# Joining the first 32-wide inverse on TensorE, with the second pair's transposes and gram products moved between the chain's stages

## What is computed

```python
k_n = k / (np.linalg.norm(k, axis=-1, keepdims=True) + 1e-06)
for t in range(S):
    y[:, :, t] = einsum('bhd,bhde->bhe', q[:, :, t], state)
    v_old = einsum('bhde,bhd->bhe', state, kt)
    state = state + bt * einsum('bhd,bhe->bhde', kt, vt - v_old)
x = y.transpose(0, 2, 1, 3).reshape(B * S, H * D)
x = (x @ w_a) * (x @ w_b) @ w_out
h = x @ w_in
out = (np.maximum(h, 0) + alpha * np.minimum(h, 0)) @ w_out2
```

## Time and profile before

| | us |
|---|---|
| median of 3 runs (lowest, highest) | 1044.02 (1043.78, 1046.03) |
| the profiled execution | 1043.06 |
| its span, first to last instruction | 1041.3 |

### The profile page before, as it was taken

How to read it: one execution, slowest core, us unless ns; L and a number is a source line. 1 busy time by engine, 2 the same in 40 slices (tenths; PEclk the granted TensorE clock), 3 DMA queues, 4 the chain that set the end, 5 groups by cost and what they waited for, 6 DMA issues and landing times.

```text
span 1041.3 us, 23976 instructions
## 1 busy us (share of the span) xinstructions
PE 1015.5 (98%) x10049; PEld 854.4 (82%) x10049; DVE 573.2 (55%) x891; ACT 405.9 (39%) x772; POOL 121.3 (12%) x126
## 2 busy tenths in 40 slices
PE   7779999999999999999999999999999999999998
PEld 6557888898888888787889788889888888888898
DVE  6967866554686343486444477544368633322433
ACT  3516445564314344413444422435431333321433
POOL 4324663450000010000001000001000000000000
PEclk9799999999999999999999999999999999999999
DMA  8827998787985566786557596556556445766662
GB/s 117 170 61 246 314 322 276 244 273 240 233 225 165 164 187 195 198 243 182 148 154 248 152 257 194 157 169 199 181 169 195 153 140 184 232 194 194 184 191 80
DMA packets 191738, 203.80 MB, mean 196 GB/s; under 512 B 109232, under 2 KB 139168, under 8 KB 191632
## 3 DMA queue, kind: packets, MB, share of 16 engines
q1 hardware_dynamic: 189040, 200.92, 65.5%
q0 software_dynamic: 896, 1.01, 0.5%
q10 hardware_dynamic: 1696, 0.34, 0.2%
HBM read 166.04 MB, written 31.46 MB: 190 GB/s over the span
## 4 chain that ended last, share of the span: by engine, by line
PE 93%; DVE 4%; issue 1%; ACT 1%; DMA 1%; POOL 0%; SPq 0%; DVEq 0%; ACTq 0%; POOLq 0%
PE bank L508 28%; PE bank L510 27%; PE bank L509 27%; PE bank L625 2%; PE bank L728 1%; PE bank L647 1%; PE bank L672 1%; PE bank L678 1%; PE bank L675 1%; PE bank L693 1%; PE bank L537 1%; PE bank L570 1%; PE bank L722 1%; PE bank L725 1%; DMA k_tok<-in_k_dram 1%
## 5 line engine op out<-in xcount | busy, mean ns | idle before, releaser
L961 ACT CAST g_hi<-g_sb 128x512 fp32r<-128x512 f32 x168 | 104.2, 620 | 246.1 <-DVE g_sb L1242 154.8
L508 PE MATMUL bank<-x_hi,w_two 128*128 128x512 f32 x432 | 171.5, 397 | 1.0 <-DVE x_lo L1231 1.0
L1247 DVE SCALAR_TENSOR_TENSOR g_sb<-f_sb,neg_alpha,e_sb 128x512 f32<-128x512 f32 x96 | 73.7, 768 | 177.5 <-ACT f_sb L958 176.9
L509 PE MATMUL bank<-x_lo,w_two 128*128 128x512 f32 x432 | 168.7, 391 | 0.0
L510 PE MATMUL bank<-x_hi,w_two 128*128 128x512 f32 x432 | 168.7, 391 | 0.0
L1253 DVE TENSOR_TENSOR g_lo<-g_sb,g_hi 128x512 fp32r<-128x512 f32 x168 | 121.1, 721 | 79.4 <-ACT g_hi L961 79.1
L510 PE MATMUL bank<-w_two,g_lo 128*128 128x384 f32 x384 | 129.5, 337 | 0.0
L508 PE MATMUL bank<-w_two,g_hi 128*128 128x384 f32 x384 | 129.4, 337 | 0.0
L509 PE MATMUL bank<-w_two,g_hi 128*128 128x384 f32 x384 | 129.0, 336 | 0.0
L1242 DVE TENSOR_TENSOR g_sb<-e_sb,bank 128x512 f32<-128x512 f32 x72 | 49.5, 687 | 136.0 <-PE bank L510 135.6
L508 PE MATMUL bank<-m_hi,w_two 128*128 128x512 f32 x288 | 118.2, 411 | 0.1
(11 more groups left out here) (153 smaller groups left out, 1543.0 us busy)
## 6 DMA issues: line engine op xcount, KB each, us to landing
w_two<-split_scratch SPq DMA_DIRECT2D x340, 384.0 KB, 3.5
split_scratch<-w_two SPq DMA_DIRECT2D x68, 384.0 KB, 4.5
w_ring<-in_moe_w_out_dram SPq DMA_DIRECT2D x28, 192.0 KB, 4.5
q_tok<-in_q_dram SPq DMA_DIRECT2D x24, 192.0 KB, 4.8
out_dram<-o_sb SPq DMA_DIRECT2D x24, 192.0 KB, 3.6
k_tok<-in_k_dram SPq DMA_DIRECT2D x23, 192.0 KB, 4.7
w_ring<-in_moe_w_in_dram SPq DMA_DIRECT2D x16, 192.0 KB, 4.2
x_raw<-y_sb SPq DMA_DIRECT2D x30, 96.0 KB, 2.4
```

The costliest lines, as they stand in the source:

```text
L508: pe.matmul(dst, lhs_hi, rhs_hi, start=start, stop=False)
L509: pe.matmul(dst, lhs_hi, rhs_lo, start=False, stop=False)
L961: act.copy(g_hi[:, j % GR], g_sb[:, j % GR]).then_inc(gh_ok, 1)
L1247: dve.scalar_tensor_tensor(g_sb[:, j % GR], f_sb[:, f % 2], neg_alpha[:, f:f + 1], e_sb[:, f % 2], ALU.mult, ALU.add).then_inc(g_ok, 1)
```

## The change

- The first inverse (pair 0) stops after the blocks of 16. A transpose X0 of half the columns goes to `dgc`, whose other half POOL has set to zero; JY multiplies it on TensorE by the gram blocks (128 products of 32 x 32 by 32 columns into banks 0 and 1), ACT copies the result to `below` (which is `prod`); JZ multiplies that by the transposed upper blocks (128 products, 16 columns); JF subtracts it in `xt` on DVE, in two parts. The transpose XT0 of the whole stands ahead of JZ. Later pairs keep the old solver.
- TR and GG of pair 1 get banks 2 and 3 of a pool of four. TR 6 and 7 and the four sets of GG move between the stages of chunks 0 and 1.
- Fillers: five, three and two around pair 0's first transposes instead of three; none between the stages up to H3 of chunk 1.
- TRK 3 and the norms (KP, KN, KI) go ahead of all four GK; BP 1 ahead of TRQ 2.
- `k_raw` of pair 1 is loaded from POOL's queue behind VS; the weights' first load waits for JF 0; the x loads are dealt out anew; GM, SQ 3, KS 3, KN 1 and KI 1 come later; the second pair's DG and solver start one unit later.

```diff
-        att, y0_bank, g0_bank = bank[6:8], bank[2:4], (bank[1], bank[4], bank[5], bank[3])
-        spare, kn_bank, b0_bank = (bank[0], bank[2]), bank[3], bank[5]
+        ab = (bank[6], bank[7], bank[0], bank[2])
+        att, y0_bank, g0_bank = ab[0:2], bank[3:5], (bank[1], bank[4], bank[5], bank[3])
+        kn_bank, b0_bank, jz_bank = bank[3], bank[5], (bank[3], ab[3])
...
-        seq += [("F", 3)] * 3 + [("KS0", 0), ("KS0", 1), ("TRK", 0), ("TRK", 1), ("TRK", 2), ("BP", 0), ("GK", 0, 0)]
-        seq += [("KS0", 2), ("KS0", 3), ("TRK", 3), ("KP",), ("KN", 0), ("KI", 0), ("GK", 1, 0), ("GK", 0, 1), ("GK", 1, 1)]
+        seq += [("F", 3)] * 5 + [("KS0", 0), ("KS0", 1), ("TRK", 0)] + [("F", 3)] * 3 + [("TRK", 1)] + [("F", 3)] * 2
+        seq += [("KS0", 2), ("KS0", 3), ("TRK", 2), ("TRK", 3), ("BP", 0), ("KP",), ("KN", 0), ("KI", 0)]
+        seq += [("GK", 0, 0), ("GK", 1, 0), ("GK", 0, 1), ("GK", 1, 1)]
...
-        for g in TR_ORDER:
-            seq += [("TR", 1, g)] + [("F", 3)] * (2 * (g >= 4))
-        for g in range(2):
-            for c in (2, 3):
-                seq += [("GG", c, g)]
-        seq += [("SQ", 2)]
-        for n in range(1, ROWS + 1):
+        seq += [("TR", 1, g) for g in TR_ORDER[0:6]]
+        for n in range(1, R16 + 1):
             seq += [("ROW", 0, n)]
-        seq += [("XT", 0)] + [("F", 0, R16 + 14)] * 3 + [("F", 0, ROWS)]
-
-        seq += [("PT", 0, 0, 0), ("PT", 0, 1, 0)]
...
+        seq += [("X0",), ("JY",), ("XT0",), ("PT", 0, 0, 0), ("PT", 0, 1, 0), ("PT", 0, 1, 1), ("JZ",), ("JF", 0), ("JF", 1)]
+
+        beside0 = {(0, "H2"): [("GG", 2, 0)], (0, "H3"): [("TR", 1, 6)], (0, "H4"): [("TR", 1, 7)],
+                   (0, "HY"): [("XL", 0, 0, T)], (1, "H1"): [("GG", 3, 0), ("PT", 1, 0, 0), ("WS", 0)],
+                   (1, "H2"): [("GG", 2, 1), ("PT", 1, 1, 0), ("WS", 1)],
+                   (1, "H3"): [("GG", 3, 1), ("PT", 1, 1, 1), ("WS", 2)],
+                   (1, "H4"): [("SQ", 2), ("KS", 2), ("WS", 3), ("WT", 0), ("WT", 1)]}
...
-                seq += [(kind, c)] + [("F", 0, 1)] * (3 * (c > 0 or kind not in ("HS", "HY"))) + beside0.get((c, kind), [])
+                seq += [(kind, c)] + [("F", 5)] * (3 * (c > 0 and kind in ("H4", "HY", "HS"))) + beside0.get((c, kind), [])
...
+        X_SP, X_ACT, X_POOL = (0, 3, 8), (1, 4), (2, 5, 6, 7, 9)
...
+                    if n == 0:
+
+                        sp.wait_ge(solve, NSOL0 - 1)
...
+                elif kind == "JY":
+
+                    pe.wait_ge(gk_free, 4)
+                    pe.wait_ge(dz_ok, 1)
+                    pe.wait_ge(solve, R16 + 2)
+                    for b in range(2):
+                        bk = in_bank(b, *st)
+                        for w in range(U):
+                            for i in range(4):
+                                mm = pe.matmul(bk[quad(i), SB * w:SB * w + SB], gs(b)[quad(i), w, SB * (i % 2):SB * (i % 2) + SB],
+                                               dgc[quad(i), U * b + w, :], start=True, stop=True)
+                        mm.then_inc(full[b], 1)
+                elif kind == "JZ":
+
+                    pe.wait_ge(gc_ok, 1)
+                    pe.wait_ge(solve, R16 + 3)
+                    for b in range(2):
+                        pe.wait_ge(*is_free(b, "JY"))
...
+                        for w in range(U):
+                            n = U * b + w
+                            for i in range(4):
+                                mm = pe.matmul(jz_bank[b][quad(i), BB * w:BB * w + BB], below[quad(i), n, :],
+                                               xt[quad(i), n, BB:SB], start=True, stop=True)
+                        mm.then_inc(jz_full, 1)
...
+                elif kind == "JY":
+                    for b in range(2):
+                        act.wait_ge(*is_full(b, *st))
+                        act.copy(below[:, U * b:U * b + U].rearrange("p w i -> p (w i)"), att[b][:, :]).then_inc(free[b], 1)
...
+                elif kind == "JF":
+                    some = slice(U * st[1], U * st[1] + U)
+                    dve.wait_ge(jz_full, st[1] + 1)
+                    dve.wait_ge(solve, R16 + 3)
+                    dve.tensor_tensor(xt[:, some, BB:SB], xt[:, some, BB:SB],
+                                      jz_bank[st[1]][:, 0:U * BB].rearrange("p (n i) -> p n i", i=BB), ALU.subtract).then_inc(solve, 1)
...
+            pool.wait_ge(solve, 1)
+            pool.memset(dgc[:, :, BB:SB], 0.0).then_inc(dz_ok, 1)
...
+                elif kind == "LK" and st[1] == 1:
+                    load_k(pool, 1, st[2], k1_ld)
```

More of the change, by code:

```diff
@@ L118, in build @@
         prod = sb("prod", [P, 2, EB * EB * EB])
+        below = prod[:].rearrange("p a b -> p (a b)").rearrange("p (n i) -> p n i", i=SB)
         mid = sb("mid", [P, 2 * EB * EB])
@@ L141, in build @@
         sq_ok, ks_ok, kn_ok, n_ok, ki_ok, v_ok = (sem(n) for n in ("sq_ok", "ks_ok", "kn_ok", "n_ok", "ki_ok", "v_ok"))
-        full, free = [sem("full0"), sem("full1")], [sem("free0"), sem("free1")]
+        full, free = [sem(f"full{b}") for b in range(4)], [sem(f"free{b}") for b in range(4)]
         y0_full, y0_free = sem("y0_full"), sem("y0_free")
         sq0_ok, ks0_ok, kp_full, b_full, b_ok = (sem(n) for n in ("sq0_ok", "ks0_ok", "kp_full", "b_full", "b_ok"))
-        sp_full, sp_free, su_ok = sem("sp_full"), sem("sp_free"), sem("su_ok")
-        sw_ok, dgp_ok = sem("sw_ok"), sem("dgp_ok")
+        su_ok, sw_ok, dgp_ok, dz_ok, jz_full = (sem(n) for n in ("su_ok", "sw_ok", "dgp_ok", "dz_ok", "jz_full"))
         gk_full, gk_free, gq_full, pt0_ok = sem("gk_full"), sem("gk_free"), sem("gq_full"), sem("pt0_ok")
@@ L263, in tile_units @@
+        seq += [("XL", 0, T, P), ("LV", 2), ("LV", 3), ("WT", 2)] + [("F", 5)] * 10 + [("XS", 0, kc) for kc in range(KC)] + [("HE", 1), ("SQ", 3), ("KS", 3), ("KN", 1), ("KI", 1)]
         def tile_units(i):
@@ L287, in beside @@
             else:
+                at[0].append(("GM", 2))
+                at[1].append(("GM", 3))
                 at[35].append(("PM", 2))
@@ L383, in build @@
         NX = len(list(x_parts()))
-        XP = [[sum(1 for n, x in enumerate(x_parts()) if x[2] == kc and (n % 3 == 2) == gp) for kc in range(KC)] for gp in range(2)]
+        X_SP, X_ACT, X_POOL = (0, 3, 8), (1, 4), (2, 5, 6, 7, 9)
+        XP = [[sum(1 for n, x in enumerate(x_parts()) if x[2] == kc and (n in X_POOL) == gp) for kc in range(KC)] for gp in range(2)]
         def x_rows(queue, p, lo, hi, some, loaded):
             yv = y_sb[:].rearrange("p (b u) s -> p b u s", b=B)
-            for h, e, kc, row, n in list(x_parts())[some]:
+            for h, e, kc, row, n in [list(x_parts())[m] for m in some]:
                 queue.dma_start(x_raw[row:row + n, kc].rearrange("p (b s) -> p b s", b=B)[:, :, lo:hi],
@@ L492, in _ @@
                         sp.wait_ge(unit_ok, NU * (p - 1) + last_ab + 1)
-                    x_rows(sp, p, lo, hi, slice(0, NX), x_ld)
+                    x_rows(sp, p, lo, hi, range(NX), x_ld)
                 elif kind == "OS":
@@ L608, in _ @@
                     for i in (2 * g, 2 * g + 1):
-                        pe.wait_ge(*is_free(i % 2, "TR", p, i))
-                        pe.wait_ge(*is_free(i % 2, "TR", p, 4 + i))
-                    if c == 3:
-                        if g == 0:
-                            pe.wait_ge(b_ok, 2)
-                        else:
-                            pe.wait_ge(sp_free, 2)
-                        bk, filled = spare, (sp_full, sp_full)
-                    else:
-                        bk, filled = in_banks(*st), full
+                        pe.wait_ge(*is_free(tr_bank(p, i), "TR", p, i))
+                        pe.wait_ge(*is_free(tr_bank(p, i), "TR", p, 4 + i))
+                    if (c, g) == (2, 0):
+                        pe.wait_ge(solve, NSOL0)
+                    two = (2, 3) if c < 4 else (0, 1)
+                    bk = [in_bank(b, *st) for b in two]
                     for j in range(UQ):
@@ L1119, in _ @@
                     dve.wait_ge(consts, MASKS)
-                    if c == 3:
-                        dve.wait_ge(sp_free, 4)
-                    else:
-                        for hf in range(2):
-                            dve.wait_ge(*is_free(hf, "GG", c, 1))
+                    for hf in range(2):
+                        dve.wait_ge(*is_free(2 + hf, "GG", c, 1))
                     dve.tensor_tensor(pt(c)[:], pt(c)[:], upper[:, 0].unsqueeze(1).to_broadcast([P, UH, T]), ALU.mult)
```

121 lines of the change are left out of this document (64 added, 57 removed).

## The result

The changed kernel takes 1048.35 us (median of five runs, 1048.1 to 1049.85). Beside it the kernel before took 1043.85 (five runs, 1041.15 to 1046.03). The ratio is 1.0047, 95% interval 1.0029 to 1.0066: slower by 0.47%, where the prediction said 1041.4 us and faster. The profiled execution took 1049.85 us, 6.8 more than the one of before.

A forecast was written before the change was run, and what follows sets the result against it. TensorE was taken as full from the first wide product (79.39 us) on, so only that start could move: -3.65 - 1.05 + 2.1 = -2.6 us, giving a median of 1041.4 us, range 1034 to 1046.5.

The forecast's parts named there:

- Opening, -3.65: Start to the solver's first transpose: fillers raise the clock at about 8 us, transpose at 16.4 instead of 20.05.
- rival of a slow opening: Opening: the clock does not rise early, so that term is +1.0 and the time 1046.0 us; chance 0.10.
- Blocks of 16 to H2, -1.05: First inverse: joining by JY and JZ, held by code fetches, takes 16.65 us instead of 17.7.
- H2 to the wide stages, +2.1: Stages of chunks 0 and 1: moved transposes, gram sets and copies cost 2.1 us; bounds -1 and +9.
- (a): Chunk 0, H2 to H3: H2 at 1.2 GHz plus a gram set, 3.5 us instead of 2.9, +0.6.
- (b): Chunk 1, H2 to H3: ScalarE's copies and a weight cast come first, 3.0 us instead of 1.9, +1.1.
- (c): Ahead of the second H4: the gram set there waits for copies likewise, +0.4 us.
- Wide stages, 0: From the first wide product on: moved GM, squares and norms cost 0, at worst 1 us, as TensorE hardly waits.
- code on time: Rival for JY and JZ: code fetches never late, products take 6.5 us, total -12.2, 1031.8 us; chance 0.13.
- The clock that stays at 1.2 GHz through the stages: Rival: clock not risen by the second H2, stages cost +6.5 us, 1047.9 us; chance 0.13.
- The rival with the clock at 2.4 GHz throughout: Rival: full clock and code blocks at 3.67 us; (a) becomes -1, JY and JZ give 0.7 more, 1038.5 us; chance 0.12.

The follow-up runs named there:

- e12: Kernel of e5 with 23 instead of four fillers between the gram sets and the first H2: 1039.2 us.
- e1: Changed kernel with 136 instead of 256 JY and JZ products, bank 1 keeping only four of each: 1045.05 us, one execution.
- e2: Changed kernel with JZ's operands in bf16, same number of products but 256 instead of 512 instructions: 1046.21 us, one execution.
- e9: Kernel of e5 plus 512 unread bf16 products on constants (1024 TensorE instructions) ahead of the first H2: 1051.88 us.
- e4: Changed kernel with only the second beta product (BP 1) put back behind GQ and GC: 1049.59 us, one execution.
- e6: Changed kernel with the second pair's squares and norms and the first GM put back where they were before: 1050.99 us, one execution.
- e7: Changed kernel with the loads of x dealt to the queues as before (four, three, three): 1049.41 us, one execution.
- e8: Changed kernel with three fillers each behind H2, H3 and H4 of chunk 0 again: 1053.09 us, one execution.
- e3: Changed kernel with the first inverse made wholly on VectorE again, so without the join: 1045.42 us, ratio to before 1.0026.
- e10: Changed kernel without the join and with norms, GM, x and k loads and BP 1 as before; opening and moved gram sets stay: 1046.87 us, ratio 1.0044.
- e5: Kernel before the change with only the new order and fillers of the opening: 1038.18 us, ratio 0.9963.
- e11: Kernel of e5 with only the second pair's norms and GM moved late as in the change: 1039.51 us, ratio to before 0.9971.
- e14: Kernel of e10 with three quarters of the second pair's gram products left out, copies and waits kept: 1045.26 us, one execution.

## Why the prediction was wrong

**Opening, -3.65: right.** The transpose was forecast at 16.4 and started at 16.3 to 16.5 in 13 of 14 experiments. In the profile of after the clock fell from about 12.3 us, and 1.5 us of the gain were lost; this execution is also the slowest of the five by 1.0 to 1.8 us. The rival of a slow opening came in part, in two of the 15 profiles (after and e12).

**Blocks of 16 to H2, -1.05: the step that failed.** It measured +3.1, 4.1 us worse. The mechanism was right: four pauses "issue" inside JY and JZ, each for one block of 256 instructions (e1, e2, e9). Two of its sizes were wrong. JY was to start "2.0 us after the blocks of 16"; it started 3.9 to 5.9 us after them (after: 4.45), since 24 transposes, 5.8 us at 1.2 GHz, stood ahead of it, behind a code pause in GQ (2.50 us at 25.09). That was read as waits for loads and copies, and its TensorE time was never added up. And JY's start to H2, forecast at 14.0 and 0.65 for the last subtraction and a handoff, was 15.3 to 16.4. In the profile of after the start of JY to the end of the first pause took 3.1 us (forecast 1.1 and 0.7), the three whole blocks, from the end of one pause to that of the next, 12.5 (forecast 11.7, from the quickest stretches), the rest 0.8 (0.5). Against 16.65 us forecast stand 20.8 in after, and 20.7 to 21.3 in e4, e6, e7 and e8, which have the whole join too. The join loses 2 to 3 us, as e3 shows.

**H2 to the wide stages, +2.1: measured +2.5, and the agreement is luck.** The places were the forecast ones, the sizes not. (a) The first H3 was to start 3.5 us behind its H2; it started 5.6 behind it (50.44 and 56.04). "I count it inside these waits" was wrong of the code: a pause of 1.55 us stands alone inside the gram set, and the set itself took 2.6 us at 1.2 GHz, not 1.8. In e3 and e10, where no pause falls there, it is 3.4. (b) In chunk 1 a gram set, ScalarE's five copies and the next gram set stand one behind the other (65.89 to 68.73); the second H3 starts 2.6 us behind its H2 (67.15 and 69.76), forecast 3.0. (c) The second H4 starts 0.9 us later behind its H3 than before, forecast 0.4. So the three places cost 4.3 us instead of 2.1, and about 1.8 came back elsewhere, in places that the forecast did not have: the pause of 1.12 us at 59.91 is gone, and the last stage's output to the first wide product takes 4.8 us instead of 5.5. Between e5 and e10, which differ in little else, the move costs 4.7 us in this stretch (27.8 to 32.5), and the old stages could do in 27.8 what took 29.9 in the profile that the forecast started from.

**Wide stages, 0: wrong by 3.4.** "TensorE hardly waits" holds for the 960 us and not for their first ten: g_sb is due there from the first unit on, and KS 3, KN, KI and GM stand ahead of it on VectorE. "0, at worst 1" was the size given; e11 shows that part alone (2.3 us more from the first wide product to the end). The wait for the second rows of x, 1.3 us, was not foreseen; e7 shows that the deal does not cause it, and e10 that it came with the moved sets.

**Together.** By the medians the opening alone gives 5.2 us (1043.33 to 1038.18), by the ratio 3.9; the moves between the stages then take back 7.2 (e3, 1045.42) to 8.7 (e10, 1046.87); the join takes 2 to 3 more. The medians of before themselves lie between 1041.4 and 1044.0 from one run to the next, so a difference of medians across runs is good to about 2 us. That e10, without the side moves, has the higher median than e3 goes with the clock: at a mean clock of 0.985 e10 takes 1043.4 to 1044.0 and e3 1045.2 to 1045.4, so the side moves cost some 1.5 us, as near as so few can tell; e11 has 1.3. Of the rivals, code on time is refuted by the four pauses and by e9. The clock that stays at 1.2 GHz through the stages came in part: in after it rose at 60.1 us, 9.7 us behind the first H2 (before: 3.1) and 1.4 behind the start of H4 of chunk 0, well ahead of the second H2, where that rival set its mark; the forecast had it in (a) only. The rival with the clock at 2.4 GHz throughout was summed wrongly: its own terms (-1 for +0.6 in (a), and 0.7) give 1039.1, not 1038.5. What share of the moved sets' cost lies with ScalarE, with code and with the clock stays open. e14, read at equal clock, puts some 5 us on the products and their code.

## What to carry to other kernels

Count instructions, not only products: in the dense runs of small products here TensorE did 256 instructions in 1.2 to 1.9 us and then stood for 2 to 3.4, so 1024 of them took 14.1 us (e9) to 16.4 (after), of which 4.9 and 6.8 were work; halving JZ's (bf16) gave 5.4. Before something is put behind a queue of an engine, add up what that queue still has to do at the clock it will have. Split a bundle of edits and time its parts: here the smallest part, the new order and fillers of the opening (not told apart), was worth 0.4% alone, and the rest gave it all back. And before a single profile is set against another, compare their mean clocks: ten executions of e10 differ by 7 us, more than most of the terms here.

## What the runs showed that was not expected

- Eleven idle products ahead of H2 instead of four shortened the stages behind it by 2.0 us (27.8 to 25.8), at a mean clock of 1.00 instead of 0.90; 23 of them held H2 for 2.2 us.
- One kernel, executed ten times, took 1043.4 to 1050.4 us in the order of its mean clock (0.985 to 0.977). So a profile with 48 of the 64 gram products gone could show a longer stretch (34.2 us at a mean clock of 0.65 instead of 32.5 at 0.88) although its execution is some 5 us shorter than those of the whole kernel at the same mean clock.
- Gains ahead of the stages did not arrive whole: in e1 the 9.4 us at H2 were 4.8 at the first wide product.
- Pauses for code came with the DMA engines otherwise idle: 2.23 us in e9, begun 0.1 us behind the start of the one code packet there.
